# A routed network's tail tiles: at most 64 tokens with both halves of each number side by side, another order on GpSimd, and the tail's code first

## The reference, cut to what matters

```python
    logits = x @ w_gate + modality_bias[modality_id]
    e_idx = np.argmax(logits, axis=1)
    ...
    for e in range(E):
        mask = e_idx == e
        ...
        h = np.maximum(x[mask] @ w1[e], 0.0)      # 512 -> 1024
        out[mask] = gate_w[mask, None] * (h @ w2[e])   # 1024 -> 512
```

## Time and profile before

| | us |
|---|---|
| median of 3 runs (1064.93 to 1065.76) | 1065.03 |
| the profiled execution | 1065.12 |
| its span, first to last instruction | 1063.4 |
| TensorE busy | 1050.7 |
| VectorE busy | 676.4 |
| ScalarE busy | 469.0 |
| POOL busy | 287.0 |

### The profile page before, as it was taken

How to read it: one execution, slowest core, us unless ns; L and a number is a source line. 1 busy time by engine, 2 the same in 40 slices (tenths; PEclk the granted TensorE clock), 3 DMA queues, 4 the chain that set the end, 5 groups by cost and what they waited for, 6 DMA issues and landing times.

```text
span 1063.4 us, 18502 instructions
## 1 busy us (share of the span) xinstructions
PE 1050.7 (99%) x5886; PEld 904.5 (85%) x5887; DVE 676.4 (64%) x1499; ACT 469.0 (44%) x975; POOL 287.0 (27%) x374
## 2 busy tenths in 40 slices
PE   8999999999999999999999999999999999999997
PEld 7999999888888888888888887888989998999996
DVE  7899999766688578758757767976662222522222
ACT  6888888745443343343343335335352222521122
POOL 6888888501000000000000000422332222223222
PEclk9999999999999999999999999999999999999999
DMA  6677688525220020002002001012381111311100
GB/s 199 204 211 214 203 254 262 175 81 159 80 80 1 1 68 12 1 0 80 1 1 80 1 1 40 5 32 90 121 277 48 52 41 40 102 59 51 46 20 22
DMA packets 57358, 90.72 MB, mean 85 GB/s; under 512 B 11470, under 2 KB 40526, under 8 KB 57168
## 3 DMA queue, kind: packets, MB, share of 16 engines
q1 hardware_dynamic: 50816, 75.17, 22.4%
q0 software_dynamic: 6208, 14.40, 4.1%
q10 hardware_dynamic: 272, 0.39, 0.2%
HBM read 70.86 MB, written 21.69 MB: 87 GB/s over the span
## 4 chain that ended last, share of the span: by engine, by line
PE 91%; POOL 3%; issue 2%; DMA 2%; DVE 1%; ACT 0%; POOLq 0%; SPq 0%; DVEq 0%; ACTq 0%
PE twin L1813 25%; PE bank L1863 13%; PE twin L1863 13%; PE twin L1935 12%; PE twin L1950 12%; PE bank L1735 5%; PE bank L1714 2%; PE twin L1702 2%; PE twin L1701 2%; PE bank L1742 2%; DMA raw_k<-k_twice 1%; POOL k_lo L650 1%; PE bank L1901 1%; PE bank L1752 1%; POOL qs L652 1%
## 5 line engine op out<-in xcount | busy, mean ns | idle before, releaser
L721 POOL DMA_INDIRECT list_scratch<-entry,slot_i x24 | 26.9, 1120 | 472.1 <-DVE slot_i L1460 460.9
L1813 PE MATMUL twin<-x_hi,w_hi 128*128 128x512 f32 x380 | 151.1, 398 | 0.0
L1813 PE MATMUL twin<-x_hi,w_lo 128*128 128x512 f32 x380 | 150.4, 396 | 0.0
L1813 PE MATMUL twin<-x_lo,w_hi 128*128 128x512 f32 x380 | 150.4, 396 | 0.0
L1586 DVE SCALAR_TENSOR_TENSOR g_lo<-twin,g_hi 128x256 fp32r<-128x256 f32 x96 | 40.7, 424 | 143.5 <-ACT g_hi L1016 140.2
L980 ACT ACTIVATE turns<-turns 128x512 f32<-128x512 f32 x96 | 60.7, 632 | 132.1 <-DVE turns L1363 130.9
L1345 DVE CUSTOM_DVE_ANT_0 whole<-y_sb,raw 128x512 f32<-128x512 f32 x160 | 109.7, 686 | 1.9
L1935 PE MATMUL twin<-xg_hi,w_hi 128*128 128x256 f32 x384 | 108.5, 283 | 0.5 <-DVE xg_lo L1486 0.5
L1935 PE MATMUL twin<-xg_lo,w_hi 128*128 128x256 f32 x384 | 108.1, 282 | 0.0
L972 ACT ACTIVATE turns<-twin 128x512 f32<-128x512 f32 x95 | 56.4, 594 | 117.2 <-PE twin L1813 117.1
L1935 PE MATMUL twin<-xg_hi,w_lo 128*128 128x256 f32 x384 | 107.2, 279 | 0.0
(11 more groups left out here) (250 smaller groups left out, 2578.8 us busy)
## 6 DMA issues: line engine op xcount, KB each, us to landing
raw<-w_expert SPq DMA_DIRECT2D x24, 512.0 KB, 6.2
raw_q<-q_twice SPq DMA_DIRECT2D x31, 384.0 KB, 3.7
raw<-w_dense SPq DMA_DIRECT2D x16, 512.0 KB, 4.5
raw_k<-k_twice SPq DMA_DIRECT2D x16, 448.0 KB, 3.8
raw_k<-k_twice SPq DMA_DIRECT2D x16, 416.0 KB, 4.7
v_sb<-v_n SPq DMA_DIRECT2D x16, 384.0 KB, 4.2
xT_scratch<-x_stage SPq DMA_DIRECT2D x16, 384.0 KB, 3.9
x_raw<-xT_scratch SPq DMA_DIRECT2D x6, 1024.0 KB, 5.4
```

The lines of the kernel that those rows point to most:

```text
L1813: last = pe.matmul(hidden_bank(c, f)[:, :], a[:, w], b[:, k, :], start=k == 0 and x == 0, stop=k == KD - 1 and x == 2)
```

## The change

The tail's limit becomes 64 entries (`TAIL`), so a last tile of 65 to 128 would be whole. `xg_hi` and `xg_lo` become views of one buffer `xg_both`, in which 64 high and 64 low columns alternate. `tail_hidden` then takes both parts of 64 tokens as one stationary operand of 128 columns, and makes two products for each block (by `w_hi` and by `w_lo`) where three stood; rows 0 to 63 of the result belong to the high part, rows 64 to 127 to the low one, and they are summed after the transpose (`add_halves`, a reduction over two), before the relu. The high and low parts of the hidden layer have 64 columns per block, and `tail_down` a stationary operand of 64 columns.

```diff
+        xg_both = sb("xg_both", [P, KD, TT // TAIL, 2, TAIL], F32R)
+        xg_hi, xg_lo = (xg_both[:, :, :, i, :] for i in range(2))
...
-            numbers(limit[:, :], [[P, NT]])
+            numbers(limit[:, :].rearrange("p (i a) -> p i a", a=2), [[TT, NT // 2], [TAIL, 2]])
...
-                        last = pe.matmul(EH_BANK[f % 2][:, 0:TT], a[:, w], b[:, k, :], start=x == 0, stop=x == 3 * KD - 1)
+                        last = pe.matmul(EH_BANK[f % 2][:, 0:TT], a[:, w], b[:, k, :, :], start=x == 0, stop=x == 3 * KD - 1)
...
-                    for x, (a, b) in enumerate(((xg_hi, w_hi), (xg_hi, w_lo), (xg_lo, w_hi))):
-                        last = pe.matmul(EH_BANK[half][:, :], a[:, k, 0:P], b[:, w], start=k == 0 and x == 0, stop=k == KD - 1 and x == 2)
+                    for x, b in enumerate((w_hi, w_lo)):
+                        last = pe.matmul(EH_BANK[half][:, :], xg_both[:, k, 0, :, :].rearrange("p h n -> p (h n)"), b[:, w], start=k == 0 and x == 0, stop=k == KD - 1 and x == 1)
...
-                    last = pe.matmul(EY_BANK[0][:, :], a[half][:, at:at + P], b[:, w], start=f == 0 and x == 0, stop=f == FB2 - 1 and x == 2)
+                    last = pe.matmul(EY_BANK[0][0:TAIL, :], a[half][:, at:at + TAIL], b[:, w], start=f == 0 and x == 0, stop=f == FB2 - 1 and x == 2)
...
-                tail_hidden(1, base, range(KD // 2))
+                tail_hidden(1, base, range(1))
                 pe.wait_ge(h_hi_made, n + 2)
                 turn_hidden(0)
-                tail_hidden(1, base, range(KD // 2, KD)).then_inc(eh_done, 2)
+                tail_hidden(1, base, range(1, KD)).then_inc(eh_done, 2)
...
-                for f in range(4, FB2 - 2):
+                for f in range(4, FB2 - 3):
```

On VectorE the tail has one instruction more for each half, and on ScalarE the second copy reads `tail_sum` in SBUF (256 columns):

```diff
+                def add_halves(half):
+                    both = TAIL_TURN[half][:, :].rearrange("p (i h n) -> p i h n", h=2, n=TAIL)
+                    dve.tensor_reduce(tail_sum[half].rearrange("p (i n) -> p i n", n=TAIL), both.rearrange("p i h n -> p i n h"), AX.X, ALU.add).then_inc(h_lo_made, 1)
...
+                dve.wait_ge(eh_done, n + 4)
+                add_halves(0)
                 dve.wait_ge(h_hi_made, n + 5)
-                dve.tensor_tensor(g_lo[0][:, :], TAIL_TURN[0][:, :], g_hi[0][:, :].bitcast(F32), ALU.subtract).then_inc(h_lo_made, 3)
+                tail_rest(0)
...
-                act.wait_ge(eh_done, n + 4)
-                act.activation(g_hi[0][:, :], TAIL_TURN[0][:, :], ACT.Copy).then_inc(h_hi_made, 3)
+                act.wait_ge(h_lo_made, n + 3)
+                act.activation(g_hi[0][:, 0:TAIL_COLS], tail_sum[0], ACT.Relu).then_inc(h_hi_made, 3)
```

POOL's loop is written anew (`prepare_rows` is `hold_entries` and `take_entries`; `fetch_rows` is the gather, the gates and the list entries):

```diff
-            with pool.Fori(1, n_tiles) as t:
-                next_rows(t)
-                for j in range(2):
-                    pool.wait_ge(scattered[j], 16 * t)
-                    pool.sem_inc(y_out_free[j], 1)
-                rows_back(t)
+            with pool.Fori(1, n_tiles - 1) as t:
+                use_entries(t + 1)
+                prepare_rows(t + 1)
+                fetch_rows(t + 1)
+                rows_back(t + 1)
+                free_rows(t + 1)
+            use_entries(n_tiles)
+            rows_back(n_tiles)
```

More of the change, by code:

```diff
@@ L178, in build_program @@
             y_sb = sb("y_sb", [P, CT, D], where=a)
-            xg_hi = sb("xg_hi", [P, KD, TT], F32R, where=a)
+            xg = sb("xg", [P, TT // P, D], where=a)
             before = sb("before", [P, P], where=a)
@@ L426, in build_program, with rows_of @@
         EH_BANK, EY_BANK, ET_BANK, FIRST_TURN = bank[0:2], bank[2:4], bank[4:6], bank[6:8]
-        TAIL_TURN = bank[6:8]
+        def rows_of(j):
+            return slice(P // TAIL * j, P // TAIL * (j + 1))
+        TAIL_TURN, TAIL_COLS = bank[6:8], D // P * TAIL
+        tail_sum = [y_sb[:, 2 + i, 0:TAIL_COLS] for i in range(2)]
         T_START, T_END, T_WHOLE, T_EXPERT, T_TILES, T_USED, T_TURNS = 0, 1, 2, 3, 4 * NE + 4, 4 * NE + 5, 4 * NE + 6
@@ L784, in next_rows, with free_rows, rows_back @@
                 load_entries(pool.value_load(tile_row[0:1, at], min_val=0, max_val=NE * N - TT))
-            def rows_back(t):
-                use_entries(t)
-                pool.drain()
+            def free_rows(n):
+                for j in range(2):
+                    pool.wait_ge(scattered[j], 16 * n)
+                    pool.sem_inc(y_out_free[j], 1)
+            def rows_back(n):
+                pool.wait_ge(now_made, 2 * n)
                 for j in (1, 0):
-                    pool.wait_ge(ey_scaled[j], t + 2)
+                    pool.wait_ge(ey_scaled[j], n + 1)
                     pool.sem_inc(carried_pool, 1)
@@ L1087, in tiles_of @@
                         tail_tile(whole_end)
[L1088 to L1097, removed]
             n_used = act.value_load(table[0:1, T_USED:T_USED + 1], min_val=1, max_val=NE)
@@ L1644, in tail_tile @@
-                splits(range(2, 4))
+                dve.tensor_copy(y_sb[:, 1, :], EH_BANK[1][:, :]).then_inc(h_lo_made, 2)
+                splits(range(2, 3))
+                dve.wait_ge(eh_done, n + 8)
+                add_halves(1)
                 dve.wait_ge(h_hi_made, n + 8)
-                dve.tensor_tensor(g_lo[1][:, :], TAIL_TURN[1][:, :], g_hi[1][:, :].bitcast(F32), ALU.subtract).then_inc(h_lo_made, 3)
-                splits(range(4, EP))
+                tail_rest(1)
+                splits(range(3, EP))
@@ L1648, in tail_tile @@
                 split_rows(t + 1, ET_BANK)
             def tiles_of(first, whole_end, last, r, parity):
-                with dve.If(first < whole_end):
+                with dve.If(first == whole_end):
+                    with dve.If(r + 1 < n_used):
+                        with dve.If(first < last):
+                            tail_tile(first, split=(r + 1, 1 - parity))
+                        with dve.Else():
+                            for f in range(EP):
+                                split_expert(r + 1, f, 1 - parity)
+                    with dve.Else():
+                        with dve.If(first < last):
+                            tail_tile(first)
@@ L1660, in tiles_of @@
                         tail_tile(whole_end)
[L1661 to L1670, removed]
             n_used = dve.value_load(table[0:1, T_USED:T_USED + 1], min_val=1, max_val=NE)
@@ L1997, in tail_tile @@
                     turn_rows(t + 1, ET_BANK)
-                for f in range(FB2 - 2, FB2):
+                for f in range(FB2 - 3, FB2):
                     tail_down(t, f, base, r)
```

61 lines of the change are left out of this document (39 added, 22 removed).

## The result

The kernel after takes 1068.77 us (median of 7 runs, 1068.74 to 1070.01), the kernel before 1065.01 beside it (7 runs): ratio 1.0038, 95% interval 1.0026 to 1.0049. It is 0.4% slower. The forecast was 1062.3 and faster.

A forecast was written before the change was run, and what follows sets the result against it. TensorE, busy 99% of the span, was taken to bound the kernel. Gains of 0.43 (first tail), 0.70 (second tail) and 1.55 (end) sum to 2.7 us, giving 1062.3 us; range 1060.6 to 1064.6.

The forecast's parts named there:

- The step that failed: Kernel's end: the 2.9 us from the last scatter's start to the span's end were to stay unchanged.
- Rival 3: Kernel's end: drain's time not saved because something else holds POOL (code behind the loop, last copies); 1063.8 us, chance 0.10.
- First tail: First tail and way into the next tile: ends 0.70 earlier, 0.45 waiting removed, part given back; worth 0.43 us.
- S: The start time of a tail's first product, from which the prediction counts its times; 890.01 in the first tail before.
- the second half's predicted 0.2 of waiting: Each tail's second half: TensorE waits 0.13 for the second transposes' chain and restarts with 0.08, 0.2 us lost.
- Second tail: Last tail: ends 0.70 us earlier, which the swapped ScalarE branches, running straight on, allow it to keep.
- The idle stretches: In a tail's first half, TensorE idles 0.66 us before the first transposes and 0.83 before the first `tail_down` product.
- The end: From TensorE's end to the last scatter: 3.55 us becomes 2.00 with the drain gone and copies earlier, saving 1.55.
- POOL's new order: POOL's queue, scatter behind a later tile's gather: nothing waits, with 4 us to spare in the last tail.
- Rival 2: ScalarE's new jumps into whole tiles cost 1.3 us like the old one: 1063.3 to 1064.6 us, chance 0.15.
- The prediction's other reading: ScalarE's new short jump, by the page prefetch rule, costs nothing to speak of; the sum would be 0.3 better.
- Rival 4: Whole tiles' 1152 products slowed by the split moving operand: 1064.1 us, chance 0.05; slower than before, chance 0.07.

The follow-up runs named there:

- a1: Kernel after with POOL's drain put back once a tile, between the next tile's list load and the wait ahead of the scatters: 1061.68 us, ratio to before 0.9969.
- a4: Kernel after with a POOL drain at the end of each loop turn, behind the waits for landed scatters: 1061.27 us, ratio to before 0.9967.
- b3: Kernel of a4 with ScalarE's and VectorE's branches in their old order, whole tiles first: 1062.68 us, ratio to before 0.9980.
- c1: Kernel of a4 with 32 unused bytes of each partition ahead of the row operands: 1047.53 us, ratio to before 0.9836.
- c3: As c1, with 96 unused bytes in place of 32: 1057.71 us, ratio to before 0.9934.
- c4: Kernel of a4 with the 32 unused bytes behind the row operands instead of ahead: 1046.67 us, ratio to before 0.9828.
- b4: Kernel before with the new tail products alone; POOL's order, its drain per tile and branches as before: 1065.92 us, ratio 1.0008.

## Why the prediction was wrong

**The step that failed** is the last sentence of the part on the end: "The last 2.9 us, from the scatter's start to the span's end, stay." They became 11.1. The prediction took the drain to be a wait whose time is saved when it goes. It was a wait and a clearing of about 0.10 us per indirect DMA since the last drain (or 0.08 for each DMA, if the list loads count too), and without it the clearing of 82 falls on the one drain that nothing hides, the closing one: +7.86 us, shown by a1 to a4. Rival 3, "the drain's time is not saved at the end", came nearest, but looked ahead of the last scatter only. Its remark that something else might hold POOL there is not what happened: the last scatter did start 2.0 us after TensorE's end. No rival had the drain's work come back later and larger.

**The sum otherwise.** The terms without this step are a gain of 2.7 us; a4 against before measured 3.6, and its 1061.27 lies in the range. The end was right; what is missing are both tails. Term by term, in the kernel after:

- *First tail, predicted 0.43 kept.* From tail to tail it is 1.09. The first `tail_down` product starts at S + 5.45 (889.42 to 894.87), predicted 5.66, and the second half's predicted 0.2 of waiting does not arise. The tail itself ends 1.20 earlier where 0.70 was said. The row split is no longer late and the next tile starts at once (901.75), as predicted. Given back up to the second tail is 0.56 of the 1.65, predicted 0.72 of 1.15. ScalarE's branch took 0.5 by itself but lengthened the chain by 0.2, predicted 0.3; and VectorE's result was followed by the third block's product within 0.06 (905.10 to 905.16), where the prediction had charged 0.2 for the release. That 0.2 was a misreading: in the earlier trace rows the product at 906.93 waits for nothing, it is TensorE's next step.
- *Second tail, predicted 0.70.* It is 1.16, for the same reasons. The idle stretches stand where they were put. In steps of 0.233 from the last start, as the prediction counts, they are 0.45 ahead of the transposes and 0.87 ahead of `tail_down` (predicted 0.66 and 0.83); the 0.28 and 0.71 in brackets are less, since they count from a modelled end. Ahead of the transposes TensorE started 0.05 after ScalarE's end (1044.66 + 0.60 to 1045.31), where 0.27 was taken from another release. That and the 0.2 of waiting in the second half are nearly all of the 0.46 that the sum missed. The reduction took 0.69 us, as taken from elementwise work on 512 elements.
- *The end, predicted 1.55.* It is 1.56, 1.99 us from TensorE's end to the scatter where 2.0 was said.
- *POOL's new order waits nowhere*: right. The last entries' copies and the empty scatter (1052.41) lie under `tail_down`.
- *Rival 2, the price of jumps*: the short jumps took 0.2 and 0.5 us and the long one 1.6, so the side taken was right. The prediction's other reading, a short jump that costs nothing, does not come out. The swap of the branches is worth 1.4 us by b3, where 0.3 to 0.6 was expected.
- *Rival 4, the split operand*: refuted. The group of line 1965 shows a mean of 282 ns in the kernel after, and its products start 0.1188 us apart on average in both kernels. The Trainium skill ("SBUF — State Buffer", Door 1: The DMA port swizzle) has full bandwidth within 16-byte lines; runs of 64 columns agree. But c1, c3 and c4 show that the place of the buffers matters to TensorE: by 3% for the 512-column products, by 1% for these.

## What to carry to other kernels

A drain in a loop is not only a wait: on POOL it also clears what DMAs leave, here 0.10 us for each indirect one, and a kernel that drops it pays for all of them at its closing drain, behind its last transfer; keep one drain a turn where the queue idles anyway and its DMAs have landed (0.46 us, hidden). Where the chain of waits ends well short of the span, read the queues' own instructions at the closing line before trusting any step that says "the rest stays". And where one part of a change needs another (here the tail needs the earlier gather and the branch order), the parts measured alone do not give the whole: the new tail alone was 1 us slower, and with its two companions the whole was 3.6 faster.

## What the runs showed of the hardware

POOL's closing drain takes 0.22 to 8.08 us by what was left undrained, while the other engines' take 8 to 455 ns in the kernel after. The Trainium skill ("VectorE: DVE Perf Modes", The DRAIN you can't avoid) calls the drains that the runtime puts ahead of and behind a program constant, about 12 ns on all engines. SyncE's 13 ns and TensorE's 8 at the kernel's own closing line are near that; ScalarE's 304, VectorE's 455 and POOL's 8,076 are not, so that figure is not to be taken for these.

In b3's profiled execution the granted clock fell from 1.00 to 0.51 for about 3 us, soon after 1.90 us in which TensorE had no products; after 1.77 and 1.74 us without any, in b4, it stayed at 1.00. That is one execution each.

The place of buffers in a partition, 32 bytes one way, changed the pace of 512-column products from 0.233 to 0.227 us at the same granted clock of 1.00, 13.5 us of the kernel before. `x_hi` at byte 173,664 and at 173,760 is slow, at 173,696 fast: these differ in whether the start is a multiple of 128, and so do the starts of the large buffers behind it (places by the order of allocation; the weights stand ahead of the pad and did not move). Whether it is that multiple, or the place against the weights, was not told apart, nor which of the operands decides. For the 256-column products of the routed stage the order is turned round: 0.1188 us with `xg_both` 32 bytes ahead of a multiple of 128 (c4), 0.1199 with it at the multiple (c1).
